# Routed rows stored in list order, and a weight ring for each half of an expert

## The chip, the cores and the metric

One Trainium2 chip, one core of it. The metric is the device time of one execution of the whole program in microseconds (us). Times are given as the median of several executions. A profiled execution gives in addition the start and the length of every instruction; its span runs from the first to the last instruction, and its own time includes what lies around the span.

The engines are named as in the profile: PE is TensorE's matmuls and PEld its weight loads, DVE is VectorE, ACT is ScalarE, POOL is GpSimd, and SP is SyncE, which here only issues DMAs.

## The reference

Three parts run in one kernel: attention with a window of 64, a dense mixture of 4 experts, and a routed layer of 8 experts with a skip. All is float32. The change is in how the third part gets its rows and weights.

```python
def _moe2_ref(x, w_skip, w_gate, w1, w2):          # N, D, E, F = 1152, 512, 8, 1024
    skip_score = x @ w_skip
    do_compute = skip_score > 0
    out = x.copy()
    xc = x[do_compute]
    logits = xc @ w_gate
    e_idx = np.argmax(logits, axis=1)
    probs = softmax(logits)
    gate_w = probs[np.arange(len(xc)), e_idx]
    for e in range(E):
        mask = e_idx == e
        h = np.maximum(xc[mask] @ w1[e], 0.0)
        y[mask] = gate_w[mask, None] * (h @ w2[e])
    out[do_compute] = xc + y
    return out

def reference(...):
    attn_out = _attn_ref(q, k, v)                  # B, H, S, D = 2, 8, 576, 64
    x = rows of attn_out                           # 1152 x 512
    x = _moe_ref(x, domain_probs, w1, w2)          # sum over 4 experts of p_e * (relu(x w1_e) w2_e)
    return _moe2_ref(x, w_skip, w_gate, u1, u2)
```

## The kernel before

**Tiles.** The 1152 rows are 9 tiles (NT) of 128 (P). Every float32 product is made as three matmuls of a high and a low part (`split_product`, `passes`), so each weight matrix has to be split: ScalarE copies a raw piece to the high part (`weights_hi`, L551), VectorE subtracts to get the low part (`weights_lo`, L702). GpSimd makes the low parts of the very first expert (L420).

**Weights.** An expert's first matrix (512 x 1024) and second matrix (1024 x 512) are each loaded in four pieces of 512 KB (`weights` in the SP block, L305) into the ring `raw`, which has RING = 4 places. A piece i is asked for when the piece before it in place i has been split: SP waits on `w1_split` or `w2_split`. SP's order is one list: first matrix, second matrix, next expert. The split weights are double-buffered in the routed part (`w1_hi[0]`, `w1_hi[1]` and so on; names with _a and _b in the trace).

**Dense part.** `dense` runs the 4 experts over three chunks of three tiles each (expert 0 over four chunks, beside the attention). Each chunk has 8 positions of hidden blocks (12 matmuls each) and 24 positions of output blocks (3 matmuls each); `beside_last` and `weight_pieces` say at which position what else is put in. The sums over experts are kept in SBUF in `x` [P, NT, D]; VectorE adds each tile to it (L824) and raises `y_added`. Beside the last expert each tile is routed (`route`: turn, logits, rank), one tile behind the sums. The result is `dest`: for each row its place in the list of its expert, or a place outside where the row is skipped; `record` holds row number and gate.

**Lists.** There is a DRAM tensor `lists` (9344 rows of 2 numbers: 8 lists of 1152 places, and 128 more) that GpSimd first fills with the number NOBODY (L408). For each tile GpSimd waits for `y_added`, stores the tile twice (`x_rows` L428 and `out` L429), waits for `dest_ready` and scatters the 128 records into `lists` with an indirect DMA (L431).

**Slots.** The routed part goes by slots of 128 places of one expert's list; with this data there are 12 slots for 8 experts (1, 2, 2, 1, 3, 1, 1, 1). The rows of slot 0 are taken out of `x` by matmuls (`take`, L1047). For each later slot GpSimd loads the 128 row numbers (`ids`, L444), gathers the rows from `x_rows` (`xg`, L448), and TensorE turns them (`turn_slot`, L1056) within the second half of the down product of the slot before. In a slot TensorE runs: up product half 0 (12 matmuls), half 1 in two parts with the turn of the hidden values between (`turn_hidden`, L1082, which waits for ScalarE's relu L624), and the down product in two halves (L1067). ScalarE then scales the output with the gate (`y_gated`, L636), and GpSimd adds it into `out` with an indirect DMA (`scatter`, L454). `around` and `finish_slot` are GpSimd's steps for each slot: scatter slot s-2, load gates, load numbers of slot s, load numbers for the scatter, gather slot s.

**Next expert's weights.** The eight pieces of the next expert are split in the first slot of the current one, at fixed points of the slot on ScalarE and VectorE: EXTRA = [(0, 1), (2,), (3,), (4,), (5,), (6, 7)]. Pieces 0 to 3 are the first matrix, 4 to 7 the second. Each engine takes its work in the order of the program, so ScalarE's relu stands behind the pieces placed ahead of it.

Of the kernel before, what the change touches and what calls it, by code (L numbers as in the profile page):

```python
# [19 lines left out]
def build_block(nc, q, k, v, dp, w1, w2, w_gate_skip, u1, u2, out):  # L20
# [87 lines left out]
    CONSTANTS = 15  # L108

# [35 lines left out]
    with ExitStack() as ctx:  # L145
# [17 lines left out]
        empty_rows = sb("empty_rows", [P, ROWS // P * 2], U32)  # L163
        slot_row = empty_rows[:, 0:P].bitcast(F32)


        sb("unused_a", [P, 120])
# [6 lines left out]
        x = sb("x", [P, NT, D])  # L174
# [23 lines left out]
        record = sb("record", [P, NT, 2], U32)  # L198
# [4 lines left out]
        ids = sb("ids", [P, 2], U32)  # L203
        gate_ids = sb("gate_ids", [P, 2], U32)
        out_ids = sb("out_ids", [P, 2], U32)
        sb("unused_b", [P, 64])
        xg = sb("xg", [P, D])
# [34 lines left out]
        x_rows = nc.dram_tensor("x_rows", (N, D), F32).ap()  # L242
        lists = nc.dram_tensor("lists", (ROWS, 2), U32).ap()
# [6 lines left out]
        raw_landed = [sem(f"raw_landed_{i}") for i in range(RING)]  # L250
        w1_hi_done, w1_split = sem("w1_hi_done"), sem("w1_split")
        w2_hi_done, w2_split = sem("w2_hi_done"), sem("w2_split")
        slot_row_made, matched, taken = sem("slot_row_made"), sem("matched"), sem("taken")
# [9 lines left out]
        lists_empty, x_stored, out_stored, listed = sem("lists_empty"), sem("x_stored"), sem("out_stored"), sem("listed")  # L263
        slots_ready = sem("slots_ready")
        ids_landed, xg_landed = sem("ids_landed"), sem("xg_landed")
        gate_ids_landed, out_ids_landed = sem("gate_ids_landed"), sem("out_ids_landed")
# [24 lines left out]
        def _(sp):  # L291
            def weights(matrix, e, before=None, pieces=range(KC)):


                for i in pieces:
# [3 lines left out]
                    dst = raw[:, i, :]  # L299
# [5 lines left out]
                    sp.dma_start(dst, src).then_inc(raw_landed[i], 16)  # L305
# [55 lines left out]
        def _(pool):  # L361
# [38 lines left out]
            step(g.iota(record[:, :, 0], pattern=[[P, NT]], base=0, channel_multiplier=1))  # L400
            step(g.memset(chosen_before[:, 0, :], 0.0))
            step(g.iota(empty_rows[:], pattern=[[0, ROWS // P * 2]], base=NOBODY, channel_multiplier=0))
# [3 lines left out]
            g.memset(xg[:], 0.0).then_inc(xg_clear, 1)  # L406
            pool.wait_ge(xg_clear, 1)
            pool.dma_start(lists.rearrange("(p n) c -> p (n c)", p=P), empty_rows[:]).then_inc(lists_empty, 16)  # L408

            for i in range(CHUNK_W):  # L410
# [7 lines left out]
                for n in range(QUARTERS):  # L418
# [3 lines left out]
            pool.wait_ge(lists_empty, 16)  # L422
            g.iota(slot_row, pattern=[[1, P]], base=0, channel_multiplier=0,
                   allow_small_or_imprecise_dtypes=True).then_inc(slot_row_made, 1)
# [735 lines left out]
```

## Time and profile before

| | |
|---|---|
| median of 3 runs | 664.93 us (664.8 to 668.19) |
| profiled execution, its own time | 669.26 us |
| its span, first to last instruction | 667.7 us |
| TensorE matmuls busy | 627.0 us (94%) |
| VectorE, ScalarE, GpSimd busy | 296.6, 247.9, 107.7 us (44%, 37%, 16%) |
| moved by DMA | 69.85 MB, mean 105 GB/s |
| granted TensorE clock, mean | 0.984 |

The page cuts the span in 40 slices of 16.7 us. TensorE is at nine tenths or more from about 50 us to about 480 us and at seven to nine tenths in the slots after it. The granted clock is nine tenths or more in all slices but the thirtieth (seven tenths) and the last. Busy time is an average: what an edit is worth must be read from the waits and the order of one stage.

### The profile page before, as it was taken

How to read it: one execution, taken by the hardware profiler on the slowest of the kernel's cores; microseconds unless marked ns; L12 is line 12 of the kernel's file. 1: busy time of each engine (PE TensorE's matmuls, PEld its weight loads, DVE VectorE, ACT ScalarE, POOL GpSimd, SP SyncE). 2: the span in 40 equal slices, each digit the busy share in tenths (PEclk: the TensorE clock that was granted, in tenths of full speed). 3: DMA queues.
4: the chain of work that ended last, by engine and by line, in shares of the span. 5: the costliest groups of instructions: out<-in, count | busy, mean ns of one | idle time of the engine just before them, and what ended most of it. 6: DMA issues, size and time to landing. Idle time of an engine off the chain costs nothing.

```text
span 667.7 us, 9826 instructions
## 1 busy us (share of the span) xinstructions
PE 627.0 (94%) x3410; PEld 557.0 (83%) x3411; DVE 296.6 (44%) x784; ACT 247.9 (37%) x518; POOL 107.7 (16%) x151
## 2 busy tenths in 40 slices
PE   5699999999999999999999999999988999899891
PEld 5598999898989898989898989899876778688671
DVE  5665566524512133512133433445673464642750
ACT  5664545421402031402031312223444475744650
POOL 7460000000000000000000011211214333234220
PEclk9999999999999999999999999999997999999996
DMA  8913143104400003400003410433475664862840
GB/s 258 270 39 109 36 135 117 48 1 127 127 0 1 1 0 127 126 0 0 0 0 126 127 63 33 99 123 86 127 204 167 215 216 146 288 200 37 281 119 7
DMA packets 42849, 69.85 MB, mean 105 GB/s; under 512 B 14927, under 2 KB 19535, under 8 KB 42816
## 3 DMA queue, kind: packets, MB, share of 16 engines
q1 hardware_dynamic: 37040, 60.73, 29.7%
q0 software_dynamic: 5776, 8.70, 5.1%
q8 instruction: 18, 0.29, 0.2%
q14 instruction: 15, 0.12, 0.1%
HBM read 63.91 MB, written 8.21 MB: 108 GB/s over the span
## 4 chain that ended last, share of the span: by engine, by line
PE 78%; DMA 8%; ACT 4%; DVE 3%; issue 2%; SPq 1%; POOL 1%; ACTq 0%; POOLq 0%; DVEq 0%
PE ps_y L993 30%; PE ps_h L993 28%; PE ps_y L1067 6%; DMA raw<-u 5%; PE ps_h L1067 4%; PE ps_o L952 2%; PE ps_s L927 2%; ACT w_hi_a L551 1%; DVE w_lo_a L702 1%; PE ps_s L972 1%; PE ps_h L1015 1%; ACT prob L570 1%; DMA raw<-w 1%; DMA ids<-lists 1%; PE ps_t L940 1%
## 5 line engine op out<-in xcount | busy, mean ns | idle before, releaser
L616 ACT ACTIVATE ht_hi<-ps_h 128x384 fp32r<-128x384 f32 (+1 forms) x104 | 48.7, 468 | 240.4 <-PE ps_h L993 231.0
L993 PE MATMUL ps_h<-xt_hi,w_hi_a 128*128 128x384 f32 (+1 forms) x400 | 131.2, 328 | 0.3 <-DVE ht_lo L808 0.3
L993 PE MATMUL ps_h<-xt_hi,w_lo_a 128*128 128x384 f32 (+1 forms) x400 | 129.4, 324 | 0.0
L993 PE MATMUL ps_h<-xt_lo,w_hi_a 128*128 128x384 f32 (+1 forms) x400 | 129.4, 323 | 0.0
L993 PE MATMUL ps_y<-w_hi_a,ht_hi 128*128 128x512 f32 x288 | 115.5, 401 | 0.3 <-POOL w_lo_a L420 0.3
L993 PE MATMUL ps_y<-w_hi_a,ht_lo 128*128 128x512 f32 x288 | 112.7, 391 | 0.0
L993 PE MATMUL ps_y<-w_lo_a,ht_hi 128*128 128x512 f32 x288 | 112.5, 390 | 0.0
L808 DVE SCALAR_TENSOR_TENSOR ht_lo<-ps_h,ht_hi 128x384 fp32r<-128x384 f32 (+1 forms) x104 | 54.8, 526 | 118.5 <-ACT ht_hi L616 118.1
L993 PEld LDWEIGHTS ps_h<-xt_hi,w_hi_a 128*128 128x128 f32 x400 | 75.5, 189 | 1.1 <-DVE ht_lo L808 0.7
L993 PEld LDWEIGHTS ps_h<-xt_lo,w_hi_a 128*128 128x128 f32 x400 | 75.4, 189 | 0.4
L993 PEld LDWEIGHTS ps_h<-xt_hi,w_lo_a 128*128 128x128 f32 x400 | 75.3, 188 | 0.0
L702 DVE TENSOR_TENSOR w_lo_a<-raw,w_hi_a 128x1024 fp32r<-128x1024 f32 x56 | 67.0, 1221 | 16.7 <-ACT w_hi_a L551 16.6
L551 ACT ACTIVATE w_hi_a<-raw 128x1024 fp32r<-128x1024 f32 x64 | 65.6, 1053 | 8.7 <-DMA raw<-u 4.7
L993 PEld LDWEIGHTS ps_y<-w_hi_a,ht_lo 128*128 128x128 f32 x288 | 54.0, 188 | 11.6
L993 PEld LDWEIGHTS ps_y<-w_hi_a,ht_hi 128*128 128x128 f32 x288 | 54.2, 188 | 10.3 <-POOL w_lo_a L420 0.6
L993 PEld LDWEIGHTS ps_y<-w_lo_a,ht_hi 128*128 128x128 f32 x288 | 54.2, 188 | 9.9
L428 POOL DMA_DIRECT2D x_rows<-x x9 | 5.2, 578 | 349.8 <-DVE x L824 349.7
L824 DVE SCALAR_TENSOR_TENSOR x<-ps_y,probs_e,x 128x512 f32<-128x512 f32 x27 | 20.3, 750 | 82.1 <-PE ps_y L993 82.1
L702 DVE TENSOR_TENSOR w_lo_b<-raw,w_hi_b 128x1024 fp32r<-128x1024 f32 x32 | 38.4, 1221 | 10.1 <-ACT w_hi_b L551 9.2
L570 ACT ACTIVATE prob<-prob,least 128x128 f32<-128x128 f32 x72 | 28.4, 395 | 36.6 <-DVE least L725 36.6
L551 ACT ACTIVATE w_hi_b<-raw 128x1024 fp32r<-128x1024 f32 x32 | 33.4, 1056 | 9.2 <-DMA raw<-u 8.8
L702 DVE TENSOR_TENSOR hs_lo<-ps_s,hs_hi 128x512 fp32r<-128x512 f32 x24 | 16.6, 690 | 42.6 <-ACT hs_hi L551 42.6
(147 smaller groups left out, 837.5 us busy)
## 6 DMA issues: line engine op xcount, KB each, us to landing
raw<-u SPq DMA_DIRECT2D x64, 512.0 KB, 4.8
raw<-w SPq DMA_DIRECT2D x32, 512.0 KB, 4.2
vt<-v SPq DMA_DIRECT2D x17, 256.0 KB, 3.1
kt<-k SPq DMA_DIRECT2D x8, 384.0 KB, 4.6
qz<-q SPq DMA_DIRECT2D x18, 128.0 KB, 3.8
x_rows<-x POOLq DMA_DIRECT2D x9, 256.0 KB, 5.0
out<-x POOLq DMA_DIRECT2D x9, 256.0 KB
kt<-k SPq DMA_DIRECT2D x1, 256.0 KB, 3.8
```

What stands on the lines that cost most here:

```text
L551: return a.activation(dst, src, ACT.Copy)
L570: a.activation(own, own, ACT.Exp, bias=least[:, u % BUFFERS:u % BUFFERS + 1], scale=-1.0, accum_out=sums[:, u % BUFFERS:u % BUFFERS + 1]). ...
L616: a.activation(ht_hi[:, pos, 0:P * tiles], ps_h[:, pos % 2, 0:P * tiles], ACT.Relu).then_inc(h_hi_done, 1)
L702: return d.tensor_tensor(dst, src, hi.bitcast(F32), ALU.subtract)
L808: d.scalar_tensor_tensor(out=ht_lo[:, pos, 0:cn], in0=ps_h[:, pos % 2, 0:cn], scalar=0.0, in1=ht_hi[:, pos, 0:cn].bitcast(F32), op0=ALU.ma ...
L824: d.scalar_tensor_tensor(out=x[:, t, :], in0=ps_y[:, t % 2, :], scalar=p_e, in1=x[:, t, :], op0=ALU.mult, op1=ALU.add).then_inc(y_added, 1)
L927: last = mm(ps_s[:, p % 2, P * half:P * half + P], qz[:, t % 3, a, half].rearrange("p j n -> p (j n)"), kt[:, t % 3, a, WINDOW * half:WIND ...
L940: last = turn(ps_t[:, P * half:P * half + P], prob[:, (2 * r + half) % BUFFERS, :], ident[:])
L952: last = mm(output_bank(r)[:, P * (2 * (r % 2) + half):P * (2 * (r % 2) + half) + P], vt[:, t % 2, half, P * a:P * a + P], prob_t[:, r % 2 ...
L972: last = mm(ps_s[:, 0, 0:E2 + 1], xr[:, c, :], w_route[:, c, :], start=(c == 0), stop=(c == KC - 1))
L993: ins = mm(dst, hi_lo[l], rhs_hi_lo[r], start=(first and n == 0), stop=(last and n == 2))
L1067: ins = mm(dst, hi_lo[l][:, b, :], rhs_hi_lo[r][b], start=(first and n == 0), stop=(last and n == len(todo) - 1))
```

## The change

Rows of `x` get two more columns, D and D + 1: the row number (written once by GpSimd) and the gate (written by VectorE). Where the records of 8 bytes were scattered, whole rows of 2056 bytes are scattered into `x_sorted`, a DRAM tensor of 9344 such rows. It is first filled with blank rows (zeros and NOBODY), by five DMAs of SP behind the loads for dense expert 1. A slot's rows, numbers and gates then come by one plain load of 128 rows that lie together; `x_rows`, its stores and the gather go. GpSimd copies the numbers out of `xg` twice per slot (`keep_ids`, `own_ids`). The nine stores of `out` move from GpSimd to SP, between weight pieces. From routed expert 2 on the second matrix has a ring of its own, `raw_more`, which lies over `x`; so its first load waits until x has been scattered, stored and taken. From expert 3 on a piece waits for the split of the same piece of the expert before it.

```diff
-        x = sb("x", [P, NT, D])
+        x = sb("x", [P, NT, D + 2])
+        raw_more = x[:].rearrange("p t d -> p (t d)")[:, 0:RING * F].rearrange("p (i f) -> p i f", i=RING)
...
-        xg = sb("xg", [P, D])
+        xg = sb("xg", [P, D + 2])
...
-        x_rows = nc.dram_tensor("x_rows", (N, D), F32).ap()
-        lists = nc.dram_tensor("lists", (ROWS, 2), U32).ap()
+        x_sorted = nc.dram_tensor("x_sorted", (ROWS, D + 2), F32).ap()
...
+            def store(t):
+                sp.wait_ge(y_added, NT * (E1 - 1) + t + 1)
+                sp.dma_start(out[P * t:P * t + P, :], x[:, t, 0:D]).then_inc(out_stored, 16)
...
-            with sp.Fori(1, E1) as e:
+            weights(w1, 1, (w2_split, 0))
+            weights(w2, 1, (w1_split, 1))
+            sp.wait_ge(xg_clear, 2)
+            blank = x_sorted.rearrange("(p n) c -> p n c", p=P)
+            for n0 in range(0, ROWS // P, BLANKS):
+                n = min(BLANKS, ROWS // P - n0)
+                sp.dma_start(blank[:, n0:n0 + n, :],
+                             xg[:].unsqueeze(1).broadcast_to([P, n, D + 2])).then_inc(rows_blank, 16)
+            with sp.Fori(2, E1) as e:
                 weights(w1, e, (w2_split, e - 1))
                 weights(w2, e, (w1_split, e))
             weights(u1, 1, (w2_split, E1 - 1))
-            weights(u1, 0, (w1_split, E1))
-            weights(u2, 0, (w1_split, E1 + 1))
+            for t in range(CT):
+                store(t)
+            for i in range(KC):
+                weights(u1, 0, (w1_split, E1), pieces=(i,))
+                if i < CT:
+                    store(CT + i)
+            for i in range(KC):
+                weights(u2, 0, (w1_split, E1 + 1), pieces=(i,))
+                if i < CT:
+                    store(2 * CT + i)
             weights(u2, 1, (w2_split, E1))
-            with sp.Fori(2, E2) as e:
-                weights(u1, e, (w2_split, e + (E1 - 1)))
-                weights(u2, e, (w1_split, e + E1))
+            weights(u1, 2, (w2_split, E1 + 1))
+            sp.wait_ge(listed, 16 * NT)
+            sp.wait_ge(out_stored, 16 * NT)
+            sp.wait_ge(xs_ready, 1)
+            weights(u2, 2, ring=raw_more, landed=more_landed)
+            with sp.Fori(3, E2) as e:
+                weights(u1, e, (w1_split, e + (E1 - 1)))
+                weights(u2, e, (w2_split, e + (E1 - 1)), ring=raw_more, landed=more_landed)
...
             for t in range(NT):
-
-                pool.wait_ge(y_added, NT * (E1 - 1) + t + 1)
-                pool.dma_start(x_rows[P * t:P * t + P, :], x[:, t, :]).then_inc(x_stored, 16)
-                pool.dma_start(out[P * t:P * t + P, :], x[:, t, :]).then_inc(out_stored, 16)
                 pool.wait_ge(dest_ready, t + 1)
-                g.indirect_dma_start(out=lists, out_offset=bass.IndirectOffsetOnAxis(dest[:, t:t + 1], 0),
-                                     in_=record[:, t, :], in_offset=None, bounds_check=E2 * LIST - 1,
+                g.indirect_dma_start(out=x_sorted, out_offset=bass.IndirectOffsetOnAxis(dest[:, t:t + 1], 0),
+                                     in_=x[:, t, :], in_offset=None, bounds_check=E2 * LIST - 1,
                                      oob_is_err=False).then_inc(listed, 16)
...
+            def load_rows(row):
+                pool.dma_start(xg[:], x_sorted[bass.ds(row, P), :]).then_inc(xg_landed, 16)
...
+            def keep_ids():
+
+                g.tensor_copy(next_ids[:], xg[:, D:D + 2].bitcast(U32)).then_inc(next_ids_kept, 1)
...
-                own = finish_slot()
-
                 pool.wait_ge(listed, 16 * NT)
-                pool.wait_ge(xg_landed, landed)
-                load_ids(ids, row, ids_landed)
+                pool.wait_ge(next_ids_kept, nth)
+                pool.wait_ge(xs_ready, later)
+                load_rows(row)
+
+                pool.wait_ge(out_stored, 16 * NT)
+                pool.wait_ge(own_ids_ready, nth)
+                pool.wait_ge(ys_gated, later)
+                scatter()
 
                 pool.wait_ge(listed, 16 * NT)
                 pool.wait_ge(scattered, landed)
-                load_ids(out_ids, own, out_ids_landed)
-
-                pool.wait_ge(x_stored, 16 * NT)
-                pool.wait_ge(xs_ready, later)
-                pool.wait_ge(ids_landed, landed_later)
-                gather()
...
+                g.tensor_copy(own_ids[:], next_ids[:]).then_inc(own_ids_ready, 1)
+
+                pool.wait_ge(listed, 16 * NT)
+                pool.wait_ge(xg_landed, landed_later)
+                pool.wait_ge(own_ids_ready, later)
+                keep_ids()
...
-                act.wait_ge(scattered, 16 * s + 16)
-                act.wait_ge(gate_ids_landed, 16 * s + 16)
+                act.wait_ge(own_ids_ready, s + 1)
                 act.wait_ge(ys_ready, s + 1)
-                a.activation(y_gated[:], ps_y[:, 0, :], ACT.Copy, scale=gate_ids[:, 1:2].bitcast(F32)
+                a.activation(y_gated[:], ps_y[:, 0, :], ACT.Copy, scale=own_ids[:, 1:2].bitcast(F32)
```

## Rows read from the trace of the kernel before

**Rows 1.** Chain that ended last, from the last list scatter: start us, us, what.
```profile
485.74 5.37 DMA lists<-record,dest
...
491.82 5.70 DMA ids<-lists
...
498.39 4.97 DMA xg<-x_rows,ids
...
503.41 1.12 PE ps_t L1056 x4
```

**Rows 2.** Waits of TensorE in 484 to 668: us in total, times, longest us.
```profile
PE ps_s L1082 <- ACT hs L624: 4.5, 3, 2.7
PE ps_t L1056 <- DMA xg<-x_rows,ids: 4.1, 1, 4.1
```

**Rows 3.** Time line of TensorE: start us, us, engine line, operation, out<-in, count.
```profile
488.78 1.21 PE L1067 MATMUL ps_h<-w_hi_a,xs_hi 128*128 128x512 f32 x4 [0.69 <-ACT xs_hi L551]
...
498.08 1.18 PE L1067 MATMUL ps_y<-w_hi_a,hs_hi 128*128 128x512 f32 x4
...
509.43 1.08 PE L1067 MATMUL ps_h<-w_lo_b,xs_hi 128*128 128x512 f32 x4
...
571.96 1.08 PE L1067 MATMUL ps_h<-w_hi_a,xs_hi 128*128 128x512 f32 x4
...
585.44 0.60 PE L1056 MATMUL ps_t<-ident,xg 128*128 128x128 f32 x4
...
587.73 1.08 PE L1067 MATMUL ps_h<-w_hi_a,xs_hi 128*128 128x512 f32 x4
588.65 1.07 PE L1067 MATMUL ps_h<-w_lo_a,xs_hi 128*128 128x512 f32 x4
...
600.09 1.08 PE L1067 MATMUL ps_h<-w_hi_a,xs_hi 128*128 128x512 f32 x4
```

**Rows 4.** Stretches: us, busy of PE, PEld, DVE, ACT, POOL, clock, DMA share, GB/s.
```profile
176.00:248.00 72.00, 72.00 (x372) 66.26 (x371) 15.18 (x26) 9.07 (x20) 0.00 (x0) 1.00 0.05 14
498.00:508.00 10.00, 5.85 (x19) 4.49 (x18) 3.65 (x4) 1.58 (x4) 5.19 (x6) 0.73 0.59 187
573.00:587.80 14.80, 11.88 (x58) 9.22 (x57) 10.27 (x11) 10.25 (x14) 4.26 (x5) 1.00 0.86 293
```

**Rows 5.** Time line of ScalarE; in brackets the idle time before it and its releaser.
```profile
488.13 0.60 ACT L551 ACTIVATE xs_hi<-ps_o 128x512 fp32r<-128x512 f32 x1 [3.79 <-PE ps_o L1047]
...
572.80 0.67 ACT L636 ACTIVATE y_gated<-ps_y,gate_ids 128x512 f32<-128x512 f32 x1
574.14 1.06 ACT L551 ACTIVATE w_hi_b<-raw 128x1024 fp32r<-128x1024 f32 x1 [0.67 <-DMA raw<-u]
577.27 1.06 ACT L551 ACTIVATE w_hi_b<-raw 128x1024 fp32r<-128x1024 f32 x1 [2.06 <-DMA raw<-u]
...
653.76 0.69 ACT L636 ACTIVATE y_gated<-ps_y,gate_ids 128x512 f32<-128x512 f32 x1 [1.25 <-PE ps_y L1067]
```

**Rows 6.** Instructions on raw in 200 to 300: ns min/median/max, first and last start.
```profile
L551 ACT ACTIVATE w_hi_a<-raw x8: 1047/1054/1055, 248.2 to 272.9; 128x1024 fp32r<-128x1024 f32 x8
```

**Rows 7.** Time line of VectorE.
```profile
154.91 2.35 DVE L702 TENSOR_TENSOR w_lo_a<-raw,w_hi_a 128x1024 fp32r<-128x1024 f32 x2
...
477.54 0.75 DVE L824 SCALAR_TENSOR_TENSOR x<-ps_y,probs_e,x 128x512 f32<-128x512 f32 x1
```

**Rows 8.** DMAs that touch out (first) and xg (second): us from issue to landing.
```profile
DMA to landing us min/median/max: 3.0/4.9/7.8
...
DMA to landing us min/median/max: 2.3/5.0/7.0
```

**Rows 9.** Time line of GpSimd.
```profile
574.41 1.64 POOL L454 DMA_INDIRECT out<-y_gated,out_ids  x1 [1.90 <-ACT y_gated L636]
```

**Rows 10.** Groups of GpSimd by form: busy us, mean ns of one, idle before it.
```profile
L402 POOL IOTA empty_rows<- 128x146 uint32 x1 | 0.3, 251 | 0.1
```

**Rows 11.** DMA in 386 to 393, two stores of 256 KB: GB/s in 40 slices.
```profile
GB/s 0 0 0 0 0 0 0 0 0 304 421 374 398 0 421 468 421 187 0 0 0 0 0 0 0 0 0 0 0 0 0 0 0 0 0 0 0 0 0 0
```

More of the change, by code:

```diff
@@ L108, in build_block @@
     CONSTANTS = 15
+    BLANKS = 16
     def beside_last(c):
@@ L250, in build_block @@
         raw_landed = [sem(f"raw_landed_{i}") for i in range(RING)]
+        more_landed = [sem(f"more_landed_{i}") for i in range(RING)]
         w1_hi_done, w1_split = sem("w1_hi_done"), sem("w1_split")
         w2_hi_done, w2_split = sem("w2_hi_done"), sem("w2_split")
-        slot_row_made, matched, taken = sem("slot_row_made"), sem("matched"), sem("taken")
+        matched, taken = sem("matched"), sem("taken")
         scores_ready, scores_masked = sem("scores_ready"), sem("scores_masked")
@@ L291, in _, with weights @@
         def _(sp):
-            def weights(matrix, e, before=None, pieces=range(KC)):
+            def weights(matrix, e, before=None, pieces=range(KC), ring=raw, landed=raw_landed):
                 for i in pieces:
@@ L528, in _ @@
             pool.reg_mov(nth, slots)
+            pool.reg_mov(later, slots + 1)
             pool.reg_mov(landed, 16 * slots)
-            pool.reg_mov(later, slots + 1)
-            pool.reg_mov(landed_later, 16 * slots + 16)
-            own = finish_slot()
+            pool.wait_ge(out_stored, 16 * NT)
+            pool.wait_ge(own_ids_ready, nth)
+            pool.wait_ge(ys_gated, later)
+            scatter()
             pool.wait_ge(listed, 16 * NT)
@@ L536, in _ @@
             pool.wait_ge(scattered, landed)
-            load_ids(out_ids, own, out_ids_landed)
-            pool.wait_ge(out_stored, 16 * NT)
-            pool.wait_ge(out_ids_landed, landed_later)
-            pool.wait_ge(ys_gated, later)
-            scatter()
-            pool.wait_ge(listed, 16 * NT)
-            pool.wait_ge(scattered, landed_later)
         @block.scalar
@@ L551, in copy, with weights_hi @@
                 return a.activation(dst, src, ACT.Copy)
-            def weights_hi(g_no, i, which):
+            def weights_hi(g_no, i, which, streamed=False):
                 j = i % KC
+                ring, landed = raw, raw_landed
                 if i < KC:
-                    h = w1_order(g_no)[1]
+                    h = g_no + (E1 + 2) if streamed else w1_order(g_no)[1]
                     dst, done = w1_hi[which][:, j, :], w1_hi_done
                 else:
-                    h = w2_order(g_no)[1]
+                    if streamed:
+                        ring, landed, h = raw_more, more_landed, g_no - (E1 + 2)
+                    else:
+                        h = w2_order(g_no)[1]
                     dst, done = w2_hi[which][:, 2 * j:2 * j + 2, :].rearrange("p j d -> p (j d)"), w2_hi_done
-                act.wait_ge(raw_landed[j], h * 16 + 16)
-                copy(dst, raw[:, j, :]).then_inc(done, 1)
+                act.wait_ge(landed[j], h * 16 + 16)
+                copy(dst, ring[:, j, :]).then_inc(done, 1)
             def attention(p):
@@ L702, in minus_hi, with weights_lo @@
                 return d.tensor_tensor(dst, src, hi.bitcast(F32), ALU.subtract)
-            def weights_lo(g_no, i, which):
+            def weights_lo(g_no, i, which, ring=raw):
                 j = i % KC
@@ L713, in weights_lo @@
                 dve.wait_ge(hi_done, n * KC + (j + 1))
-                minus_hi(lo, raw[:, j, :], hi).then_inc(split, 1)
+                minus_hi(lo, ring[:, j, :], hi).then_inc(split, 1)
             def attention(p):
```

85 lines of the change are left out of this document (30 added, 55 removed).

## Prediction

> **What bounds the kernel now.** I read the chain of waits first: until 484 us it is matmuls, nearly without a gap, and what the change puts in there must be hidden, not fast. After that come the twelve slots of the routed experts. There the chain leaves TensorE for two things: three DMA latencies in a row before the first gathered slot [rows 1], and waits of TensorE for ScalarE [rows 2]. The time line of TensorE shows the size: a slot without loads takes 12.36 us (587.73 to 600.09), slot 6, which splits the next expert's weights right after another slot that did so, takes 15.77 (571.96 to 587.73) [rows 3], the longest wait for a relu, 2.7, in it [rows 2]. ScalarE's time line names the cause of that hole: it sat 2.06 us for a weight piece still under way, and the relu behind it on ScalarE came late [rows 5]. A ring of four pieces means that piece 4 of an expert is only asked for when piece 0 has been split.
>
> Books of the stage: first slot begins at 488.78 [rows 3], the last result is scaled at 653.76 [rows 5], so 164.98 us for 12 slots; 12 x 12.36 = 148.3; 16.7 us are lost. Of these 4.15 are TensorE's wait for the first gathered rows [rows 2]. After it the granted clock of the stretch 498 to 508 is 0.73 [rows 4], that is part of it at 1.2 GHz instead of 2.4: from the turn at 503.41 [rows 1] to the third matmul group behind it at 509.43 are 6.02 us, where slot 6 takes 3.21 for the same instructions (585.44 to 588.65) [rows 3]. That is 2.8 us. The other 9.7 are late weight pieces and small gaps.
>
> **Part 1, rows in list order.** Removed on the path: last list scatter 5.37, load of numbers 5.70, gather 4.97, each with some 0.6 to 0.7 of issue ahead [rows 1]. Put in: the last scatter now carries rows of 2056 B instead of 8 B; behind it one plain load. The scatter still starts at 485.74, since it waits for the same index. It isn't in the trace; nearest rows are the scatters into the output (3.0 to 7.8, median 4.9) and the transfers touching xg or the stored rows (2.3 to 7.0, median 5.0) [rows 8], and the list scatter itself, 5.37. I take 5.9: the list's 5.37 and 0.5 for 128 rows that must be moved. The load takes 5.7 + 0.5 = 6.2 in the same manner. So rows are in SBUF at 485.74 + 5.9 + 0.7 + 6.2 = 498.5. TensorE asks for them four matmuls after 498.08, at 499.0 [rows 3]. The wait of 4.15 goes, and with it the idle time ahead of the low clock: 4.15 + 2.8 = 6.95. With both at their longest (7.8 and 7.0) they land at 501.2, and 2.2 of the wait stays, perhaps with the clock loss; with both at their shortest nothing more is gained.
>
> The first numbers and gates come by a second small load, issued 0.6 later, about 498.8; they are needed at the first slot's scaling, about 501.3. Per slot GpSimd loses three loads of numbers (0.55 to 1.2 us of issue each) and a gather and gets one load and two copies of 128x2. The copy is not in the trace: nearest is a fill of 146 columns at 0.25 us [rows 10], an upper bound for two columns if only data counts; with its semaphore I take 0.3. Each sits behind a landing (scatter, or rows) where a load of numbers (5.70 in [rows 1]) stood before, so scaling is asked for no later. Scatter of slot s-2 is issued at slot start + 2.4 (574.41 against 571.96) [rows 9, 3], lands by +10.2 at worst [rows 8], and its numbers are needed at +12.4: 1.9 us of cover in the worst case, about 5 in the usual one. The row load is now queued ahead of that scatter on GpSimd, but its wait (the turn) ends before the scaling does, and it costs 0.6 of issue. All this is costed at nothing; if the cover is gone it is 1:1 per slot.
> The Trainium skill (GPSIMD Engine Reference, Specifications) says that GpSimd shares its SBUF interfaces with VectorE and contends with VectorE instructions that have two SBUF inputs. The weight subtracts are such. By it a copy could wait out one subtract; the cover above takes it, so the sum stays. No row here shows such a wait.
>
> **Part 2, a ring for each half.** With eight places the pieces of expert e+2 are asked for when those of e+1 are split, a slot or more ahead (12.4 us) instead of half a slot. ScalarE's waits for DMA then end. Two neighbouring one-slot experts ask for 4.19 MB of weights; with rows in and out 4.72 MB. In 573 to 587.8 the queues moved 293 GB/s at a share of 0.86, so 341 at full share [rows 4]: 13.8 us. That is over one slot, but never more than two such slots follow each other with loads left, and the eight places are full at the start of each pair, so it is covered.
> What is late next is ScalarE itself. In slot 6 its scaling comes at 572.80 and the first weight piece at 574.14 [rows 5], 2.2 after the slot's start, of which 0.67 was a wait for DMA. Two pieces at 1.0 and the relu of 0.6 end at +4.5; TensorE wants the relu at +4.1 (12 + 6 matmuls at 0.23). So 0.4 stays in slot 6 and in slot 10, the two that follow a splitting slot. For slot 1 the second ring fills only after slot 0's last split: six pieces (3.1 MB) from about 500 on take 9.2 us + 3 of latency, to 512, when ScalarE wants the last: I leave 0.3. The first slot is 0.2 longer than the others, and 0.1 rounding at the end. Of 9.7 there stay 0.8 + 0.3 + 0.2 + 0.1 = 1.4, so 8.3 goes.
> The second ring lies over x, so its first load waits for the last scatter (491.7), the stores and the first rows taken (488): all before 500, when SP gets there. Nothing is queued behind that wait but loads that come later anyway.
>
> **Part 3, stores moved to SP.** Nine stores go from GpSimd's queue to SP's, and x's own copy goes altogether. Behind store(8), whose sum is ready at 478.3 [rows 7], waits one weight piece; with 5 to 6 us it lands at 483.5 to 484.5. ScalarE splits it last before the first rows and then sat idle for 3.79 until 488.13 [rows 5]; a late piece eats of that. Nothing. Before, GpSimd was free of its stores when each index came, so its scatters start no earlier now.
>
> **Part 4, blanks.** 9344 rows x 2056 B = 19.2 MB written by SP behind the last load of expert 1's second half, issued when the subtracts at 154.91 are done, 157.3 [rows 7]. Expert 2's first half is queued behind it and ScalarE wants it from 248.2 on [rows 6]. Cover: 90.9 us in which the queues move 14 GB/s [rows 4]. At 341 GB/s the fill takes 56 us; two stores beside each other moved at 374 to 468 GB/s in their full slices [rows 11], which gives 48; paid as single stores of 0.26 MB at 2.3 us each [rows 8] it is 114 GB/s, 169 us. I take 56, since these are queued transfers of 4.2 MB. Cost nothing.
> The Trainium skill (DMA: Bandwidth & Descriptors, How a descriptor splits into AXI transactions) says that a row that doesn't start on a 256-byte boundary is fetched from the boundary below. A row of 2056 B then costs up to 2560: 70 us instead of 56. That speaks against this row width, and is still inside the cover. No row here shows such a row width.
>
> **Sum.** 6.95 + 8.3 = 15.25 off the profiled execution: 669.26 - 15.3 = 654.0 (span 667.7 to 652.4; what lies around it stays). That execution is 4.3 above the median; of the three runs two are at 664.9 and one at 668.2, 3.3 apart, near the size of the clock loss. I read this as a loss of clock that comes in some executions and not in the median one: 664.93 - 12.5 = 652.4. Were it in the median too: 649.7. I predict 652.0.
>
> **Rivals.** (a) Rows still late, both transfers as long as the longest rows: 2.2 to 5 us of the gain stay out, 654 to 657. For it: the scatter moves far more bytes. Against: medians. 0.12. (b) Weight loads still bind, the 341 GB/s being the limit: part 2's gain mostly stays out, 657 to 660. For it: 13.8 against 12.36; against: the reserve of a full ring. 0.14. (c) Slower: the fill outlasts its cover. TensorE first feels it when VectorE, stuck behind the late split, misses the sum of tile 6, about 258 (248.2 + 15 positions at 0.69), so the point is 19.2 + 1.0 MB in 101 us: below 200 GB/s. At the 114 GB/s above the fill ends at 326 and two pieces at 329: 71 us of stall, 723. For it: rows of odd width, never seen here. Against: all rates of queued transfers in the rows. 0.08. (d) Little happens, some new wait on GpSimd per slot eats the gain, 662 to 670: 0.07. Forecast, 649.5 to 654.5: 0.59.
>
> The range: from 649 to 660 holds the forecast, (a) and (b), some 0.83. Faster by over 0.5% (about what a measurement can tell): 0.86; within: 0.05; slower: 0.09.
>
> **What would show it.** Right: no wait of the first turn for xg and a granted clock near 1.00 in that stretch; ScalarE's weight copies without waits for DMA; slots 6 and 10 at 12.8 us; the fill at 157 to about 215 with TensorE whole until 478. Wrong: a second wait for rows or numbers in the slots, copies on GpSimd that take over a microsecond, a gap of TensorE at 250 to 275.

## The result and the profile after

The changed kernel takes 649.43 us (median of 6 runs, 647.97 to 650.19); beside it the kernel before took 666.08 (6 runs, 664.8 to 668.19). The ratio is 0.9722, interval 0.9694 to 0.975. A later comparison gave 649.05 and 0.9732 (0.9701 to 0.9763). The forecast was 652.0 with a range from 649 to 660: right in sign, 2.6 us too slow, and at the range's edge. By ratio, 0.9722 stands against 652.0 / 664.93 = 0.9805, which is outside the interval: 0.9722 of 664.93 would be 646.4, below the range.

The profiled execution took 648.53 us, its span is 646.9. From its page: engine totals, then GB/s in 40 slices of the span, and two DMA groups (count, KB each, median us to landing).

```profile
PE 622.0 (96%) x3410; PEld 555.7 (86%) x3411; DVE 297.4 (46%) x784; ACT 246.6 (38%) x518; POOL 76.3 (12%) x119
...
GB/s 262 264 54 86 62 97 91 124 1 150 223 262 232 254 241 198 92 61 0 0 0 70 106 100 60 13 136 75 97 158 209 358 216 248 211 360 54 199 129 9
...
x_sorted<-xg SPq DMA_DIRECT2D x4, 4112.0 KB, 44.7
...
x_sorted<-xg SPq DMA_DIRECT2D x1, 2313.0 KB, 43.5
```

Then the waits in 460 to 647 (us in total, times, longest), which answer to [rows 2]. All that is left for TensorE in the slots is the last line here, 0.2; the wait for xg and the relu waits are gone. ScalarE's waits for weights are 0.7 and 0.2.

```profile
POOL own_ids L499 <- DMA out<-y_gated,own_ids: 49.0, 11, 6.7
...
ACT w_hi_a L557 <- DMA raw<-u: 0.7, 1, 0.7
...
PE ps_s L1088 <- ACT hs L634: 0.2, 1, 0.2
```

TensorE's time line, from the first slot to the first turn of gathered rows, and ScalarE's last scaling:

```profile
488.61 1.18 PE L1073 MATMUL ps_h<-w_hi_a,xs_hi 128*128 128x512 f32 x4 [0.69 <-ACT xs_hi L557]
...
497.85 1.09 PE L1073 MATMUL ps_y<-w_hi_a,hs_hi 128*128 128x512 f32 x4
498.78 0.60 PE L1062 MATMUL ps_t<-ident,xg 128*128 128x128 f32 x4
499.13 1.17 PE L1073 MATMUL ps_y<-w_lo_a,hs_hi 128*128 128x512 f32 x4
```

```profile
637.37 0.69 ACT L645 ACTIVATE y_gated<-ps_y,own_ids 128x512 f32<-128x512 f32 x1 [1.30 <-PE ps_y L1073]
```

Three stretches on these two time lines close the books. To the first slot: 488.61, before 488.78, so 0.2 less. First slot to last scaling: 148.76, before 164.98, so 16.2 less. From there to the span's end: 646.9 - 637.37 = 9.5, before 667.7 - 653.76 = 13.9, so 4.4 less. Together 20.8, the difference of the spans. These are the stretches of two single executions; a second execution of the kernel before has 158.9 in the middle stretch (below). The forecast had 15.25 in the second stretch and nothing in the third.

The windows (start:end us, length, busy of PE, PEld, DVE, ACT, POOL, clock, DMA share, GB/s), against [rows 4]: the clock of 498 to 508 is 1.00 where it was 0.73; in slot 6 and during the fill the DMA engines are full.

```profile
165.00:240.00 75.00, 75.00 (x390) 69.31 (x389) 20.48 (x31) 13.64 (x24) 0.00 (x0) 1.00 1.06 240
498.00:508.00 10.00, 10.00 (x50) 8.27 (x49) 7.03 (x7) 6.34 (x9) 2.22 (x2) 1.00 0.83 281
563.30:575.60 12.30, 12.30 (x62) 10.17 (x61) 11.23 (x12) 10.88 (x15) 2.97 (x3) 1.00 0.98 356
```

GpSimd's time line answers to [rows 1] and [rows 9]: scatter, load of rows, load of numbers, copies; then the same in slot 6.

```profile
485.57 0.98 POOL L456 DMA_INDIRECT x_sorted<-x,dest  x1 [6.39 <-DVE dest L783]
489.37 0.60 POOL L467 DMA_DIRECT2D xg<-x_sorted  x1 [2.82 <-DMA x_sorted<-x,dest]
489.95 0.57 POOL L517 DMA_DIRECT2D next_ids<-x_sorted  x1
493.60 0.89 POOL L519 COPY own_ids<-next_ids 128x2 uint32<-128x2 uint32 x1 [3.07 <-DMA next_ids<-x_sorted]
494.62 0.19 POOL L477 COPY next_ids<-xg 128x2 uint32<-128x2 uint32 x1
...
565.51 1.61 POOL L471 DMA_INDIRECT out<-y_gated,own_ids  x1 [2.67 <-ACT y_gated L645]
573.52 1.17 POOL L499 COPY own_ids<-next_ids 128x2 uint32<-128x2 uint32 x1 [6.41 <-DMA out<-y_gated,own_ids]
```

The rows are in SBUF when the second copy starts, at 494.62 at the latest; by the trace's record of the load's semaphore they landed at 493.4. That is 5.4 us before TensorE asks, and 5.1 us earlier than the 498.5 of the forecast.

### The profile page after: what moved, and what is told of

Same layout as the page of the kernel before. It is cut to its first block, busy times and chain, and to the rows that moved or that the text cites. A ratio compares the mean times of both kernels' runs of the same rounds, so it can differ in the third digit from the quotient of the medians.

```text
span 646.9 us, 9656 instructions
## 1 busy us (share of the span) xinstructions
PE 622.0 (96%) x3410; PEld 555.7 (86%) x3411; DVE 297.4 (46%) x784; ACT 246.6 (38%) x518; POOL 76.3 (12%) x119
## 4 chain that ended last, share of the span: by engine, by line
PE 90%; DMA 2%; ACT 2%; DVE 2%; issue 1%; SPq 1%; POOL 1%; DVEq 0%; POOLq 0%; ACTq 0%
PE ps_y L999 31%; PE ps_h L999 29%; PE ps_y L1073 9%; PE ps_h L1073 9%; PE ps_o L958 2%; PE ps_s L933 2%; PE ps_s L1088 2%; PE ps_s L978 1%; PE ps_t L946 1%; DMA raw<-u 1%; PE ps_o L1053 1%; DMA raw<-w 1%; PE ps_h L1021 1%; PE ps_t L1062 1%; ACT prob L580 1%
## 5 line engine op out<-in xcount | busy, mean ns | idle before, releaser
L711 DVE TENSOR_TENSOR w_lo_a<-raw,w_hi_a 128x1024 fp32r<-128x1024 f32 x44 | 52.9, 1222 | 15.1 <-ACT w_hi_a L557 15.0
L456 POOL DMA_INDIRECT x_sorted<-x,dest x9 | 9.2, 1026 | 429.2 <-issue 345.4
L557 ACT ACTIVATE w_hi_a<-raw 128x1024 fp32r<-128x1024 f32 x52 | 53.2, 1051 | 4.8 <-PE ps_y L999 1.8
L933 PE MATMUL ps_s<-kt,qz 128*128 128x128 f32 x144 | 25.4, 309 | 6.2 <-DMA kt<-k 6.2
L933 PEld LDWEIGHTS ps_s<-kt,qz 128*128 128x128 f32 x144 | 23.4, 222 | 7.2 <-issue 5.8
## 6 DMA issues: line engine op xcount, KB each, us to landing
x_sorted<-xg SPq DMA_DIRECT2D x1, 2313.0 KB, 43.5
```

What stands on the lines that cost most here:

```text
L456: g.indirect_dma_start(out=x_sorted, out_offset=bass.IndirectOffsetOnAxis(dest[:, t:t + 1], 0), in_=x[:, t, :], in_offset=None, bounds_che ...
L557: return a.activation(dst, src, ACT.Copy)
L711: return d.tensor_tensor(dst, src, hi.bitcast(F32), ALU.subtract)
L933: last = mm(ps_s[:, p % 2, P * half:P * half + P], qz[:, t % 3, a, half].rearrange("p j n -> p (j n)"), kt[:, t % 3, a, WINDOW * half:WIND ...
```

## Experiments

**The two parts apart.** First the rows in list order with the old ring of four.

```diff
-            weights(u1, 2, (w2_split, E1 + 1))
-            ...
-            weights(u2, 2, ring=raw_more, landed=more_landed)
-            with sp.Fori(3, E2) as e:
-                weights(u1, e, (w1_split, e + (E1 - 1)))
-                weights(u2, e, (w2_split, e + (E1 - 1)), ring=raw_more, landed=more_landed)
+            with sp.Fori(2, E2) as e:
+                weights(u1, e, (w2_split, e + (E1 - 1)))
+                weights(u2, e, (w1_split, e + E1))
```

> Rows in list order kept, second ring taken away. If the gain of the ring is what the books say (9.7 us of late weight pieces, of which the changed kernel keeps 0.5), the routed stage from the first slot's matmuls to the last scaling grows from 148.8 to 158 us, with ScalarE waiting for DMA in slots 6, 9 and 10, and this kernel is 9 us slower than the changed one and 8 to 12 faster than before. Rival: with the rows early the pieces are early enough in one ring too, because the first loads are asked for 6 us sooner; then it is within 2 us of the changed kernel.

Measured 657.15 us (654.45 to 657.98), ratio 0.9847 (0.9798 to 0.9896); span 654.9. From the first slot (489.30) to the last scaling (645.62) it takes 156.3 us, where 158 was expected and the change has 148.8. Waits in 460 to 660: TensorE has none for xg, but those for late weight pieces are back.

```profile
ACT w_hi_b L551 <- DMA raw<-u: 6.7, 7, 1.5
...
PE ps_s L1082 <- ACT hs L628: 3.5, 2, 2.1
...
PE ps_y L1067 <- ACT hs_hi L551: 2.8, 4, 1.3
```

Then the kernel before with the second ring alone, laid over x as in the change.

```diff
+            weights(u1, 2, (w2_split, E1 + 1))
+            sp.wait_ge(x_stored, 16 * NT)
+            sp.wait_ge(out_stored, 16 * NT)
+            sp.wait_ge(xs_ready, 1)
+            weights(u2, 2, ring=raw_more, landed=more_landed)
```

> The kernel before with the second ring alone: numbers, gather and stores stay as they were. Books: 8.3 to 9.2 us off, the wait for the first gathered rows and the stretch at the lower clock stay; 656 to 659 us against 666. Rival: GpSimd's chain of three loads per slot now gets in the way, because the queues are fuller, and waits for gathered rows or for gates appear in later slots; then less than 6 us are gained. GpSimd's last DRAIN stays at 7.4 us if it goes by the number of its DMAs (90 here).

Measured 659.07 (657.86 to 661.59), ratio 0.9876 (0.9833 to 0.9918); span 660.0. Waits in 460 to 665, and a window of slot 1:

```profile
ACT y_gated L648 <- DMA gate_ids<-lists: 5.2, 1, 5.2
...
PE ps_t L1068 <- DMA xg<-x_rows,ids: 2.6, 1, 2.6
PE ps_s L1094 <- ACT hs L636: 2.1, 1, 2.1
...
ACT w_hi_b L559 <- DMA raw<-u: 0.2, 1, 0.2
```

```profile
498.00:518.00 20.00, 15.26 (x59) 11.87 (x58) 8.84 (x9) 8.66 (x12) 8.47 (x9) 0.83 0.85 276
```

The wait for rows stays, the clock falls behind it, and the first scaling waits for its gates; that holds back the relu of slot 1. The load of these gates took 6.9 us from issue to landing, against 4.0 and 5.1 in the two executions of the kernel before; the DMA engines' share in 503 to 508 was 0.98, against 0.32 and 0.22. That the weights of the second ring delay it is argued from this and was not tested alone. Each part therefore removes its own waits. By medians against the 666.6 of the same comparison, part 1 took off 9.5 (interval 6.9 to 13.5) and part 2 took off 7.5 (5.5 to 11.1), together 17.0; the whole change takes off 16.7 to 18.3 in its two comparisons. So the sizes add up, within a few microseconds. Of part 1's 9.5, some 4.5 are in the tail: from the last scaling to the span's end it has 9.3, the second ring alone has 14.0.

**The tail.** The idle time after the last scatter is no instruction of a view. In the trace's own records it is one DRAIN of GpSimd, an instruction of its sequencer that ends the program. Counted from those records:

```
kernel                     DMAs issued by GpSimd   last DRAIN, us
before                     90                      7.425
before, again              90                      7.425
second ring alone          90                      7.425
after                      34                      2.849
rows late (below)          36                      3.012
56 more DMAs (below)       90                      7.422
drains added (below)       34                      0.137
```

To see whether the count sets it, 56 tiny stores by GpSimd were put into the dense part, at a time when it has nothing else to do: they were issued between 47 and 109 us, over 500 us before the end.

```diff
+            for n in range(56):
+                pool.dma_start(notes[n, 0:128], y_gated[0:128, 0:2]).then_inc(noted, 16)
+                if n % 8 == 7:
+                    pool.wait_ge(noted, 16 * (n + 1))
```

> The changed kernel with 56 more small stores (128 rows of 8 B) issued by GpSimd in the dense part, where it is idle, so that it issues 90 as the kernel before does. If GpSimd's last DRAIN goes by the number of its DMAs since the start, it grows from 2.85 to 7.4 us and the span by 4.6 us, with nothing else changed. Rival: it goes by what was issued last (gathers and loads of numbers before, others after), then it stays at 2.85.

Measured 651.68, one execution, span 650.1; no wait in the slots. Its last scaling:

```profile
636.24 0.69 ACT L651 ACTIVATE y_gated<-ps_y,own_ids 128x512 f32<-128x512 f32 x1 [1.31 <-PE ps_y L1079]
```

So 13.9 us follow it, the figure of the kernel before, and the stretch from the first slot (487.94) to it is 148.3 us, as after (148.8). The slope is (7.422 - 2.849) / 56 = 0.082 us for each DMA that GpSimd issued, and the kernel with 36 fits it: two more DMAs, 0.163 more. What the DRAIN does with them the records don't tell.

If the last DRAIN goes through what has gathered since the one before, drains in the middle, where GpSimd waits anyway, take it off the end.

```diff
+                if t == NT - 2:
+                    g.drain()
...
                 keep_ids()
+                g.drain()
```

> The changed kernel with a drain on GpSimd after the eighth row scatter and at the end of each slot's steps, where GpSimd waits anyway. If the last DRAIN works off what GpSimd's DMAs left since the drain before (82 ns each), it falls from 2.85 us to 0.1 to 0.3 and the kernel takes 2.6 us less, about 646.8. If each DRAIN costs by the number of DMAs since the program's start, the last stays at 2.85 and the ones in the slots grow from 0.7 to 2.8 us each, which makes the row loads late only in slots where GpSimd is short of time; then no gain or a loss of up to 2 us.

Measured 646.24 (645.58 to 646.99), ratio 0.9674 (0.9637 to 0.971); span 643.7. The last DRAIN takes 0.137, and the last scaling, at 636.83, is followed by 6.9 us instead of 9.5. The drains in the slots take 0.43 to 1.6 us each. Part of that is the copy that GpSimd is still at: they end 0.24 to 0.25 us after that copy where two DMAs were issued since the drain before, and 0.50 us after it in the first of these slots, where it was five. One DMA before the last drain left 0.137. A fixed 0.07 and 0.082 for each DMA would give 0.23, 0.48 and 0.15, so the count since the drain before is what matters. The drain behind the next to last row scatter takes 6.3; it ended 0.4 us after that scatter had landed (483.7 and 484.1; in the second execution of this kernel 483.9 and 484.3), so it waited for it. That the drains cost nothing shows in GpSimd's time line: the load of rows behind slot 6's copies is issued at 576.04, 87.6 us after the first slot began, against 87.8 in the changed kernel.

```profile
572.63 0.39 POOL L501 COPY own_ids<-next_ids 128x2 uint32<-128x2 uint32 x1 [6.03 <-DMA out<-y_gated,own_ids]
573.18 0.98 POOL L479 COPY next_ids<-xg 128x2 uint32<-128x2 uint32 x1 [0.16 <-POOL own_ids L501]
576.04 0.57 POOL L469 DMA_DIRECT2D xg<-x_sorted  x1 [1.88 <-issue]
```

The same kernel once more, beside the change itself:

> The kernel with drains once more, beside the changed one: 2.7 us faster by the last DRAIN (0.14 instead of 2.85), so 646.7 against 649.4, ratio of the two 0.996, if nothing in the slots waits for the drains put there.

> The changed kernel once more, beside the kernel with drains on the same chip: 649.4 us, ratio to before 0.972 to 0.975, first slot begins within 1.5 us of 488.6, last DRAIN 2.85 us.

Measured 646.25 (645.38 to 647.08) against 649.05 (648.29 to 649.65): 2.8 us less, the 2.7 of the DRAIN. This version is the fastest of the study.

**What late rows cost.** Two loads of numbers, one after the other, were put ahead of the first load of rows, so that rival (a) happens.

```diff
+            pool.dma_start(next_ids[:], x_sorted[0:P, D:D + 2].bitcast(U32)).then_inc(delayed, 16)
+            pool.wait_ge(delayed, 16)
+            pool.dma_start(next_ids[:], x_sorted[0:P, D:D + 2].bitcast(U32)).then_inc(delayed, 16)
+            pool.wait_ge(delayed, 32)
             load_rows(row_1)
```

> The changed kernel with two small loads in a row put ahead of the first row load, each waited for. They took about 3.6 us each in the changed kernel, so rows land about 7 us later, near 501.5, and TensorE waits 2 to 3.5 us for them. If the wait brings on the lower clock, the stage grows by the wait and by up to 2.8 more: 3 to 6 us in all, and a stretch at 0.5 shows after the wait. Rival: the clock only falls after a longer idle time, then the stage grows by the wait alone, 2 to 3.5.

Measured 653.95 (652.95 to 655.16), ratio 0.98; span 653.2. The chain that ended last (start, us, what), TensorE's wait, and two windows:

```profile
487.65 3.31 DMA x_sorted<-x,dest
...
491.25 3.62 DMA next_ids<-x_sorted
...
495.15 3.27 DMA next_ids<-x_sorted
...
499.10 4.64 DMA xg<-x_sorted
```

```profile
PE ps_t L1067 <- DMA xg<-x_sorted: 2.7, 1, 2.7
```

```profile
498.00:508.00 10.00, 7.33 (x30) 5.64 (x29) 4.07 (x5) 2.78 (x5) 1.97 (x5) 0.83 0.88 277
504.40:507.60 3.20, 3.20 (x9) 2.47 (x8) 0.69 (x1) 0.60 (x1) 0.73 (x2) 0.50 0.91 301
```

A delay of 7.9 us (491.25 to 499.10) puts the rows 2.7 us too late, and the first slot to the last scaling (490.70 to 643.61) grows from 148.76 to 152.91, by 4.15: the wait of 2.7, and 1.5 for the matmuls that then run at half clock. So the change has about 5 us of slack here, and this wait cost one and a half times its length.

**The clock in the kernel before.** The prediction took the low clock for something that only some executions have.

> The kernel before once more, for a second profile of it and the granted clock and span of each run. The prediction read its 4 us between profiled execution and median as a loss of clock that comes in some executions only. Then the runs fall into groups about 2.8 us apart, with mean clocks of about 0.984 and 0.989 or more, and a profile near the median shows the stretch after the wait for the first gathered rows at the full clock. Rival: the clock is lost in every execution, and the spread comes from the start of the kernel or the length of DMA waits.

Measured 666.96 (12 runs, 663.57 to 669.59). The profiled one was the shortest of the twelve, and it has the loss as well:

```profile
PE ps_t L1056 <- DMA xg<-x_rows,ids: 2.0, 1, 2.0
```

```profile
498.00:508.00 10.00, 8.02 (x31) 6.17 (x30) 3.45 (x5) 3.09 (x5) 4.51 (x6) 0.83 0.57 187
502.00:505.30 3.30, 3.30 (x9) 2.53 (x8) 0.69 (x1) 0.36 (x1) 0.76 (x2) 0.50 0.59 216
```

Here the wait is 2.0 instead of 4.15, and the clock is at half for 3.4 us instead of 6.8 (502.6 to 509.4 in the first profile). From the first slot to the last scaling this execution takes 158.9 where the first took 164.98. The twelve times lie spread over the 6 us, with no gap of 2.8 between two groups. Two of the twelve have a mean clock of 0.991 and 0.992, which leaves 11 to 12 us at half clock, about what the stretch behind the last scaling takes alone in the two profiles (10 to 12); these two may have been without the loss. They took 668.19 and 665.86 and are not the shortest, so the loss is not what parts the short executions from the long ones.

**The fill.** Its five transfers in the changed kernel (issue ns min/median/max, first and last start):

```profile
L361 SPq DMA_DIRECT2D x_sorted<-xg x5: 469/16122/19344, 157.5 to 199.9; - x5
...
DMA to landing us min/median/max: 24.4/43.5/53.3
```

The last starts at 199.9 and lands 43.5 later, at 243.4: 85.9 us, 224 GB/s, where 56 us were forecast. Expert 2's first piece is split from 248.0 on, so of 35 us of reserve 4 were left. In four other profiled executions with this fill it took 81.7 to 83.2 us. Three kernels repeat the fill, into a spare tile, during expert 2's window, with other row lengths and other pitches (the pitch is the distance from the start of one row to the start of the next). ROW stands for the row's length in numbers, 512 or 514.

```diff
+            extra = spare.rearrange("(p n) c -> p n c", p=P)
+            for n0 in range(0, ROWS // P, BLANKS):
+                n = min(BLANKS, ROWS // P - n0)
+                sp.dma_start(extra[:, n0:n0 + n, 0:ROW],
+                             xg[:, 0:ROW].unsqueeze(1).broadcast_to([P, n, ROW])).then_inc(spared, 16)
```

Rows of 2048 B, one behind the other:

> The changed kernel with a second fill beside dense expert 2, behind that expert's loads, of a spare tensor with rows of 2048 B (19.1 MB). The fill of 2056-byte rows moved 248 GB/s at a full DMA share. If the odd row is what slows it, the second fill moves at 340 or more and is over in 56 us; if stores of this size just run at some 250 GB/s, it takes 76 to 78 us like the first. The span stays within 2 us of the changed kernel in either case, since expert 3's first half is wanted 90 us after it begins.

The same 2048 B, but each row starts 2056 B behind the last:

> As the run with rows of 2048 B, but these rows stand 2056 B apart in DRAM, so only the start of each row is odd, not its length. If the start on no 256-byte boundary costs (each row then touches one more block), it is slow like the first fill, 250 GB/s; if it is the 8 bytes left over at a row's end, it is as fast as rows of 2048 B that lie together.

Rows of 2056 B, each starting 2304 B behind the last:

> As the run with rows of 2048 B, but the spare tensor has rows of 2056 B that stand 2304 B apart, so that each starts on a 256-byte boundary and has 8 bytes left over at its end. If only the start matters, it takes about 54 to 60 us for 19.2 MB like the aligned rows; if the odd end costs as well, it lies between 60 and 80.

Their lines, in this order; each is a group of issues followed by the landing times, then the window 262 to 300 of each.

```profile
L370 SPq DMA_DIRECT2D spare<-xg x5: 462/10163/10709, 257.6 to 286.2; - x5
...
DMA to landing us min/median/max: 15.7/25.4/28.8
```

```profile
L370 SPq DMA_DIRECT2D spare<-xg x5: 462/15249/16368, 259.2 to 298.4; - x5
...
DMA to landing us min/median/max: 22.1/40.3/45.6
```

```profile
L370 SPq DMA_DIRECT2D spare<-xg x5: 461/10834/11070, 258.1 to 287.3; - x5
...
DMA to landing us min/median/max: 15.8/27.7/31.7
```

```profile
262.00:300.00 38.00, 38.00 (x195) 34.77 (x194) 12.09 (x17) 8.23 (x13) 0.00 (x0) 1.00 1.04 397
```

```profile
262.00:300.00 38.00, 38.00 (x194) 34.53 (x193) 12.01 (x16) 7.73 (x12) 0.00 (x0) 1.00 1.06 271
```

```profile
262.00:300.00 38.00, 38.00 (x195) 34.61 (x194) 12.01 (x16) 7.73 (x12) 0.00 (x0) 1.00 1.06 378
```

The fills end a median landing after their last issue, as above: 53.9, 79.5 and 56.9 us. The pitch decides, not the length: 2048 B at a pitch of 2056 cost 1.47 times those at 2048, and 2056 B at a pitch of 2304 cost 1.06 times. Each is one execution, and the same fill varied by 5% above, so the 1.06 may be nothing. The pitches 2048 and 2304 are multiples of 256 and 2056 is not; which boundary counts these three don't tell. All three kernels have TensorE whole (spans 647.0 to 648.5), so the odd pitch costs cover and not time.
The Trainium skill (DMA: Bandwidth & Descriptors, How a descriptor splits into AXI transactions) says that a descriptor that doesn't start on a 256-byte boundary begins at the boundary below, and that the bytes before its start still cost beats. The runs agree that such rows cost more when written to DRAM, and they cost more than this counting gives: at most 248 bytes are added to a row of 2048, a factor of 1.12 by our estimate from the page, and 1.47 was measured.

Rival (c) needs a fill that outlasts its cover. Four more transfers of 4.2 MB, directly behind the first five, make one.

```diff
+            extra = spare.rearrange("(p n) c -> p n c", p=P)
+            for n0 in range(0, 4 * BLANKS, BLANKS):
+                sp.dma_start(extra[:, n0:n0 + BLANKS, :],
+                             xg[:].unsqueeze(1).broadcast_to([P, BLANKS, D + 2])).then_inc(spared, 16)
```

> The changed kernel with four more transfers of 4.21 MB behind the fill, 16.8 MB. At 248 GB/s the fill ends 68 us later, about 311; expert 2's first pieces land about 315 instead of 244. TensorE should stand from about 258 to 318: span 646.9 + 57 to 62, with the stall in one piece, and a spell at the lower clock behind it. Rival: SP alone is held up, and the weights' pieces overtake the fill in the 16 queues, then the span grows by less than 20 us.

Measured 697.24, one execution, span 695.7, 48.8 above that of after. ScalarE's time line, and TensorE's only wait in 200 to 330:

```profile
301.25 1.06 ACT L564 ACTIVATE w_hi_a<-raw 128x1024 fp32r<-128x1024 f32 x1 [51.98 <-DMA raw<-w]
```

```profile
PE ps_y L1006 <- DVE x L837: 45.8, 1, 45.8
```

The wait is where the prediction put it, for VectorE's sum behind the late split, and begins at 259.7, after the last matmuls that need no sum. The stall is less than the 57 to 62 expected: fills and first pieces, 37 MB, went from 157.5 to 301.2 at 257 GB/s, where the fill alone had 224. Of the other 3 us some 1.7 are the matmuls at half clock behind the stall (from 305.51 to 309.02 eight of 0.23 us take 3.5); the rest is open. Rival (c)'s mechanism is thus real. It is kept off by 4 us before ScalarE would wait, and by about 11 us before TensorE would: by the landing records the first piece came 57.1 us later than in the changed kernel (301.23 against 244.17), and TensorE stood 45.8.

## Why the prediction was right and where it was wrong

**Right.** Three latencies ahead of the first gathered slot, the low clock behind them and ScalarE's late pieces were what could be gained in the slots. The wait (4.15) and its clock loss (2.8) are gone to the last tenth: TensorE's turn at 498.78 waits for nothing and the clock is 1.00. The stores on SP and the fill hide, as said. The gap that only the fill could make appears at its forecast place when the fill is made longer.

**The step that failed: "what lies around it stays".** The forecast kept the 13.9 us behind the last scaling, as if it were the cost of one scatter. 4.4 of them went. The prediction gave no reason for keeping them; it put this term at nothing. They belong to GpSimd's last DRAIN, which grows by 0.082 us with each DMA that GpSimd issues; the change takes that count from 90 to 34 and the DRAIN from 7.4 to 2.8. The rows had a hint: a scatter into the output has a median of 4.9 us [rows 8], its issue takes 1.6 [rows 9], and 13.9 minus these left 7 us that the sum never named. It is the largest miss, of the size of the whole error in the profiled span (5.5 = 4.4 + 1.0 in the ring + 0.2 before the first slot; rounding 0.1).

**The way to the median: size near, reason wrong.** I took 2.8 out, reading the low clock as absent from the median execution. It is in the shortest of twelve too, so its absence is not what makes an execution short. Its length and the waits for DMAs differ, and the profiled 669.26 is 2.3 above the median of twelve. By the runs, the stage's gain by medians is 17.0 - 4.5 = 12.5 (the two parts apart), the 12.5 that the prediction subtracted. But it subtracted it from 664.93, a median of three, where twelve give 666.96. Forecast 652.0, tail -4.4, start value +2.0: 649.6, against 649.43 measured; with the 666.08 of the comparison itself as start value it would be 648.8. The two errors had opposite signs. That the measured median lies inside the stated range at all was luck: 16.7 us went, where 12.9 were forecast.

**Ring: 9.3 instead of 8.3.** I left 0.4 each to slots 6 and 10, 0.3 to slot 1. Slot 6 takes 12.32 (563.31 to 575.63 on TensorE's time line). ScalarE's time line shows why:

```profile
563.89 0.68 ACT L645 ACTIVATE y_gated<-ps_y,own_ids 128x512 f32<-128x512 f32 x1
564.46 2.01 ACT L557 ACTIVATE w_hi_b<-raw 128x1024 fp32r<-128x1024 f32 x2
566.36 0.59 ACT L634 ACTIVATE hs<-ps_h 128x512 f32<-128x512 f32 x1
```

The sum had a slip here: 2.2 less the wait of 0.67, two pieces at 1.0 and the relu of 0.6 make 4.1, which is when TensorE wants it, and not 4.5. By its own terms the sum should have left nothing in these two slots, and the ring would have come to 9.1. In the trace it is better still: from the start of the scaling to the first piece it takes 0.57, where [rows 5] have 1.34 with the wait in it, and the relu begins at +3.0 and ends at +3.6. Slot 1's wait for its pieces was 0.7 and 0.2, as sized, but TensorE feels 0.2 of it at most. All this is for the profiled execution of the kernel before. In its shortest execution (158.9 for the stretch, with a wait of 2.0 and some 1.7 of clock loss) the same books leave 6.5 for the ring, so a single pair of executions doesn't fix this term to 1 us.

**Fill: 86 us instead of 56.** The rate of 341 GB/s came from loads with rows in and out [rows 4], its bound from stores without the odd pitch [rows 11], and the rows of 2056 B start anywhere. The cost of nothing came true with 4 us to spare for ScalarE and 11 for TensorE, not with 35. This was luck in a term that I gave a chance of 0.08. The 70 us for the odd row width had an error as well. By the counting of the Trainium skill (DMA: Bandwidth & Descriptors, How a descriptor splits into AXI transactions) a row of 2056 B that starts up to 248 B behind a boundary costs at most 2304 B and not 2560, by our estimate 63 us and not 70. The fill took 86.

**Scatter of rows: 3.1 instead of 5.9.** The last row scatter was issued at 485.57 and landed, by the record of its semaphore, at 488.62, though it moves 257 times the bytes. The nine of the changed kernel took 2.6 to 5.4. I had started from the list scatter's 5.37. The load took 4.0 instead of 6.2. Both misses are harmless, since slack isn't time; they are the reason why rival (a) was further off than 0.12. Rival (b) did not happen: DMA share 0.98 in slot 6, and TensorE whole.

**Copies on GpSimd: 0.18 to 1.19 instead of 0.3.** With the long ones, the numbers of slot 6 were there at 574.7, 1 us before its end, where I had 1.9 of cover in the worst case. The long ones end when a weight subtract of VectorE does: copy 573.52 to 574.69, subtracts 572.30 to 574.65; copy 493.60 to 494.49, subtract 493.22 to 494.45. The short one at 494.62 lies beside a subtract that reads PSUM. All 24 copies sort this way: the seven long ones begin while a weight subtract runs and end within 0.05 us of its end, the others took 0.18 to 0.19. The prediction named copies of over a microsecond as a sign of being wrong; two came (1.17 and 1.19), and TensorE waited for neither.
The Trainium skill (GPSIMD Engine Reference, Specifications) says that GpSimd's SBUF interfaces are shared with VectorE. It names VectorE instructions with two SBUF inputs, and the trace agrees; no run here took the VectorE work away, so the cause is argued and not shown.

## What to carry to other kernels

Name every microsecond of the profiled span before you call any of it fixed. The stretch behind the last result is part of the kernel, and here 7 of its 14 us hung on how many DMAs one engine had issued. Where a step is declared hidden, give its duration both by the nearest rate and by the worst layout of its bytes: here 35 us of reserve shrank to 4, and a longer fill made the kernel slower than it was before. A stall of TensorE cost more than its length here, so a chain of DMAs ahead of a matmul is worth removing to the point of slack and not beyond: 5 us of it were left unused here.

## What the runs showed of the hardware

- A DRAIN of GpSimd takes 0.07 us and 0.082 for each DMA that GpSimd has issued since the drain before (1: 0.137, 34: 2.849, 36: 3.012, 90: 7.42), even where 56 of them ran over 500 us earlier. Drains in between take it off the end, for 0.43 to 1.6 us each, part of it a copy under way. One that met a scatter under way took 6.3 us and ended 0.4 us after the landing.
- Stores from SBUF to DRAM moved 397 GB/s with rows of 2048 B, 378 with 2056 B at a pitch of 2304, and 271 with 2048 B at a pitch of 2056. DMA share was above 1.0 in all three. One execution each.
- SP was held up for 0.5 us by the first issue of such a transfer of 4.2 MB, for 6 to 7 by the second and for 10 to 19 by each later one, while the ones ahead were under way; what stands behind them in its program waits that long.
- After TensorE waited 2.0 to 4.15 us for rows, the granted clock fell to half (0.50, 1.2 GHz) for 3.4 to 6.8 us. In the changed kernel there is no such wait and no such stretch in the slots.
- A copy of 128x2 elements on GpSimd took 0.18 us, and 0.76 to 1.19 us where it began beside a weight subtract of VectorE (profile of the changed kernel).
